# Turning, taking and summing the later units' queries one step later in an attention and two-layer kernel

## The reference

```python
# q, k, v: (4, 8, 576, 64); pooled attention over means of 4 tokens, plus a banded local attention
q_d, k_d, v_d = means of 4 neighbouring tokens
out_up = repeat(softmax(q_d k_d^T / 8) v_d, 4)
out_local = softmax(where(|i - j| < 4, q k^T / 8, -1e9)) v
x = (out_up + out_local) as (2304 tokens, 512)
g = s * max(x @ w_in, 0)**2 + b        # 512 x 2048
x = g @ w_out                          # 2048 x 512
out = ((x @ w_a) * (x @ w_b)) @ w_out2 # 512 x 1536, 1536 x 512
```

## Time and profile before

| what | value |
|---|---|
| time, median of 3 runs | 975.58 us (975.18 to 975.60) |
| the profiled execution's own time | 975.64 us |
| its span, first to last instruction | 973.8 us |
| TensorE matmuls, busy | 951.3 us (98% of the span) |
| VectorE, ScalarE, GpSimd, busy | 611.1, 474.5, 202.0 us (63%, 49%, 21%) |
| granted TensorE clock, mean | 0.984 |
| DMA, mean over the span | 73 GB/s |

### The profile page before, as it was taken

How to read it: one execution, slowest core, us unless ns; L and a number is a source line. 1 busy time by engine, 2 the same in 40 slices (tenths; PEclk the granted TensorE clock), 3 DMA queues, 4 the chain that set the end, 5 groups by cost and what they waited for, 6 DMA issues and landing times.

```text
span 973.8 us, 18322 instructions
## 1 busy us (share of the span) xinstructions
PE 951.3 (98%) x6902; PEld 898.5 (92%) x6902; DVE 611.1 (63%) x1087; ACT 474.5 (49%) x1112; POOL 202.0 (21%) x216
## 2 busy tenths in 40 slices
PE   6899999999999999999999999999999999999997
PEld 5799999999999999999999999999999999999996
DVE  5788655655555556555547666666856667766642
ACT  4677554545554445454434544444634345644432
POOL 2200211001210011200012033333333333333310
PEclk8599999999999999999999999999999999999999
DMA  8346220111300122101041142222442222422201
GB/s 199 104 136 164 65 59 20 45 45 43 88 21 20 48 64 67 44 19 44 14 154 34 50 137 66 66 66 66 135 143 79 67 66 66 130 66 65 75 24 66
DMA packets 129352, 71.41 MB, mean 73 GB/s; under 512 B 63248, under 2 KB 120304, under 8 KB 129264
## 3 DMA queue, kind: packets, MB, share of 16 engines
q1 hardware_dynamic: 128224, 69.94, 25.0%
q10 hardware_dynamic: 1040, 0.29, 0.1%
HBM read 60.76 MB, written 9.44 MB: 72 GB/s over the span
## 4 chain that ended last, share of the span: by engine, by line
PE 88%; ACT 6%; DVE 3%; issue 2%; DMA 1%; SPq 1%; POOL 0%; ACTq 0%; DVEq 0%
PE bank L736 27%; PE bank L686 19%; PE bank L672 18%; PE bank L752 15%; ACT sml L795 3%; PE bank L572 2%; PE bank L636 2%; PE bank L619 1%; PE bank L629 1%; PE bank L548 1%; DMA natk<-in_k 1%; ACT smp L786 1%; PE bank L603 1%; PE bank L566 1%; ACT kT L774 1%
## 5 line engine op out<-in xcount | busy, mean ns | idle before, releaser
L736 PE MATMUL bank<-wx 128*128 128x384 f32 x1512 | 287.4, 336 | 0.6 <-ACT u L977 0.6
L736 PEld LDWEIGHTS bank<-wx 128*128 128x128 f32 x1512 | 267.1, 188 | 14.6 <-ACT u L977 0.9
L686 PE MATMUL bank<-g_hi,wx 128*128 128x288 f32 x1024 | 232.1, 302 | 0.0
L672 PE MATMUL bank<-wx 128*128 128x288 f32 x1536 | 226.9, 296 | 0.5 <-ACT relu L889 0.5
L672 PEld LDWEIGHTS bank<-wx 128*128 128x128 f32 x1536 | 211.7, 189 | 0.7 <-ACT relu L889 0.7
L1236 POOL TENSOR_TENSOR raw<-raw 128x256 f32<-128x256 f32 x144 | 143.3, 1013 | 302.9 <-DVE wx L1156 263.4
L686 PEld LDWEIGHTS bank<-g_hi,wx 128*128 128x128 f32 x1024 | 171.4, 188 | 5.3 <-issue 5.2
L752 PE MATMUL bank<-wx 128*128 128x512 f32 x648 | 173.4, 394 | 0.8 <-DVE wx L1156 0.8
L686 PE MATMUL bank<-g_lo,wx 128*128 128x288 f32 x512 | 151.5, 296 | 0.0
L752 PEld LDWEIGHTS bank<-wx 128*128 128x128 f32 x648 | 119.3, 188 | 17.2 <-DVE wx L1156 1.5
L1112 DVE SCALAR_TENSOR_TENSOR g_lo<-relu,b_col,g_hi 128x288 fp32r<-128x288 f32 x128 | 70.6, 552 | 80.4 <-ACT g_hi L894 80.4
(11 more groups left out here) (70 smaller groups left out, 858.8 us busy)
## 6 DMA issues: line engine op xcount, KB each, us to landing
raw<-in_moe_w_b SPq DMA_DIRECT2D x72, 128.0 KB, 2.3
raw<-in_moe_w_a SPq DMA_DIRECT2D x72, 128.0 KB, 2.3
raw<-in_moe_w_out SPq DMA_DIRECT2D x36, 256.0 KB, 2.8
vnat<-in_v SPq DMA_DIRECT2D x32, 144.0 KB
o_transposed<-o_sb SPq DMA_DIRECT2D x8, 576.0 KB, 3.4
o_raw<-o_transposed SPq DMA_DIRECT2D x6, 768.0 KB, 6.3
out<-y SPq DMA_DIRECT2D x18, 256.0 KB, 2.3
natq<-in_q SPq DMA_DIRECT2D x63, 72.0 KB, 2.1
```

The lines of the kernel that those rows point to most:

```text
L672: mm = nc.tensor.matmul(HB[:, 0:HALF], wi(w, kd, f), xs(x, c % 2)[:, kd], start=(kd == 0 and j == 0), stop=(kd == KD - 1 and j == 2))
L686: mm = nc.tensor.matmul(ACC[o][:, 0:HALF], wo(w, f, o), g[:, slot % GB, :], start=(f == 0 and j == 0), stop=(f == F1 - 1 and j == 2))
L736: mm = nc.tensor.matmul(dst, left(w, n, a, kd), right(x, i)[:, kd * HC:(kd + 1) * HC], start=(opens and kd == 0 and m == 0), stop=(kd == K ...
```

## The change

`turn_q` and `take_q` of units 4 to 31 go from tick -4 to tick -3, `sum_q` from tick -3 to tick -2. The alone units keep their ticks. No instruction, wait or buffer is added or taken away.

```diff
@@ TensorE
-                for u in at_tick(g, 1, -4, TURN_SKEW):
+                for u in at_tick(g, 1, -3, TURN_SKEW):
                     turn_q(u)
@@ VectorE
-                for u in at_tick(g, 2, -3, TURN_SKEW):
+                for u in at_tick(g, 2, -2, TURN_SKEW):
                     sum_q(u)
```

## The result

| | before | with the change |
|---|---|---|
| median | 975.38 us (974.59 to 975.60, 4 runs) | 987.86 us (987.70 to 988.27, 4 runs) |
| ratio | | 1.013 (95% interval 1.0113 to 1.0148) |
| span of the profiled execution | 973.8 us | 985.9 us |

A forecast was written before the change was run, and what follows sets the result against it. TensorE's list was taken to bound the kernel, its matmuls busy for 951.3 of 973.8 us. The terms -3.7 + 5.0 + 4.7 + 1.2 + 1.2 = +8.4 us on 975.6 us gave 984.0 us, range 980.8 to 988.5.

The forecast's parts named there:

- The clock: Rival, 8%: after chunk 0's waits of 2.3 us TensorE falls to 1.2 GHz, 4.2 us a fall: 988.2 or 992.4 us.
- Part 1: Leading units: `turn_q` no longer waits for `take_k`, 0.34 us at each of 11 waits, -3.7 us; no new stall.
- called by 0.06 us: Unit 18, which leads: TensorE reaches `turn_local` at 260.97, where 260.91 would do, so no stall.
- Part 2: Units 12 to 15, 20 to 23, 28 to 31: `turn_local` newly waits 0.42 us each for `take_q`, +5.0 us.
- Part 3: Chunk 0: `take_q` behind two splits of weights delays `turn_local`; units 6 and 7 +4.7 us, unit 8 +1.2 us.
- the short waits vanish inside that one: Unit 8: TensorE's short waits for the keys' transfer and `take_k` vanish, since ScalarE sets the end.
- Part 4: Units 4 and 5: later `take_q` and `sum_q` delay `scores`, then `turn_local`; +1.2 us together, bounds +0.5 and +2.4.
- Against it: the waits are short, and the matmuls before them unbroken: Argument against a fall to 1.2 GHz after chunk 0's waits of 2.3 us; that rival got 8%.
- a low digit in the page's clock row: Sign that the forecast is wrong: the changed kernel's clock row has a low digit behind the second slice.
- the forecast's second ground for it: Transposes, which follow each long wait, do not count as work for TensorE's clock, by the Trainium skill.
- nothing waits: Rival, 6%: `turn_local` finds the queries taken at every unit, only the leading units' gain is left: 971.9 us.
- long waits are handed back: Rival, 6%: waits of 2.35 us in units 6 and 7 spare TensorE later waits, taking off 4.7 us: 979.3 us.

The follow-up runs named there:

- the run filled with transposes: The change plus 22 extra transposes of the identity ahead of `turn_local` of units 5, 6 and 7, results not used: 984.27 us.
- the filled kernel: The change plus 13 extra matmuls into the free bank 1 ahead of `turn_local` of units 5, 6 and 7, results not used: 984.05 us.
- only leading units late: Against the kernel before, `turn_q`, `take_q` and `sum_q` one tick later for the 11 leading units only (9 to 11, 16 to 19, 24 to 27): 971.66 us.
- ahead of the splits: The change with `take_q` of units 5 to 8 on ScalarE behind `split_g_hi` but ahead of the two splits of weights: 978.53 us.

## Why the prediction was right, and where it was short

The direction, the mechanism and the four parts of the sum held. The clock, which had no term in the sum, did not.

- **Part 1, leading units: right.** -3.7 us was forecast; -3.96 by slots, -4.2 in the kernel that has nothing else. The stall was put at 0.34 us, it was 0.36. That no new stall follows there was called by 0.06 us; none shows.
- **Part 2, units that don't lead: right.** +5.0 forecast, +5.07 by slots, 0.42 each as taken.
- **Part 3, the waits of chunk 0: right in size.** 4.7 + 1.2 = 5.9 forecast; 5.75 once the clock is held up. The long part of them is the two splits of weights, as the kernel with `take_q` ahead of them shows. By slots the three cost 2.26, 1.65 and 1.83 us, not 2.35, 2.35 and 1.2. `turn_local` is held as long at unit 7 as at unit 6 (86.62 - 82.60 = 4.02 us from the start of its up group, against 66.82 - 62.79 = 4.03), but some of that comes back before unit 8: the 0.38 us that TensorE waited for the transfer of unit 8's keys, at 91.37, are gone, and the wait for unit 8's queries is longer by as much and more. The forecast had said that the short waits vanish inside that one, so the sum of the two, 3.48 us, is what it gave (3.55).
- **Part 4, units 4 and 5: right, hidden by chance in the table.** +1.2 forecast. From unit 3's `values` (L629) to the third up group it was 50.37 - 38.35 = 12.02 us and is now 50.91 - 37.79 = 13.12, so +1.10. The other profiles repeat this: 12.02 to 12.03 in the four kernels that start as before or move only TensorE's turning there, 13.11 in the four that start as the change does. In the change's profiled execution the start came to L629 0.56 us sooner, hence +0.55 in the table; over the ten profiles that moment lies anywhere from 37.60 to 38.54.
- **The clock: wrong.** This is the step "Against it: the waits are short, and the matmuls before them unbroken". The fall was priced as a rival at 8% and left out of the sum. It came after all three long waits, unit 8's of 1.7 us too, and cost 4.63 us in all, 1.5 us for each. The rival's own price of 4.2 us a fall was too high: I took four groups of matmuls at the low clock, and each low stretch of 3.42 us has room for 1.2 groups of 2.79 us. No row of the trace before had an idle time of this length at full clock, and absence of a row was read as evidence. The forecast's sign for it, a low digit in the page's clock row, could not have shown it either: three stretches of 3.42 us leave every slice of 24.6 us at a 9. The rule of the Trainium skill ("TensorE: Matmul & The Clock Gate", "HAM oscillation — how this bites in real kernels") that idle gaps between bursts lower the clock, which the forecast weighed and did not follow, was the better guide. The trace agrees with it in direction only: the waits in the page's example are longer than the 1.67 to 2.20 us here, and the forecast's second ground for it, that transposes don't count, failed in the run filled with transposes.

The measured 12.5 us are then -3.96 + 5.07 + 5.75 + 1.10 + 4.63 = 12.6. Without the clock it would be 8.0, where the sum had 8.4. That the time still fell inside the range is luck: the range was wide enough for it because it added up high bounds of parts that came out near their middle, not because it foresaw three falls.

The rival *nothing waits* (971.9 us) fell for the change as made, and gives the time of the kernel in which only TensorE's turning is late, 971.77 us, to 0.1 us. The rival *long waits are handed back* fell: the filled kernel keeps 5.75 us of them in slots 4 to 16, and slots 16 to the end show no gain beyond the leading units'.

## What to carry to other kernels

When a step is moved on several engines at once, ask for each whether the move serves anything there: here TensorE's move alone brings 4 us. ScalarE's copy and VectorE's sum, moved along with it, cost 16 us; by the waits most of that is the copy's, which lands behind work that finishes late. Before a copy is put later, compare the tail of what it will stand behind with the moment its reader arrives; two engines that meet within 0.1 us are one small shift away from a stall. And price an idle time of TensorE of 2 us twice: once as a wait, once for the clock.

## What the runs showed of the hardware that was not expected

Waits of 1.67, 2.18 and 2.20 us on a TensorE that had been at full clock for the 17 to 20 us before the fall were each followed by a stretch of 3.42 us at 1.2 GHz, which began 0.2 to 1.5 us after the work had resumed, and so slowed work rather than idle time. Waits of 1.39 and 1.40 us were not, and 2 us of transposes in the same place held the clock up as matmuls did.

In the start the clock rises at different times in kernels whose code is the same there. With only leading units late, whose start is instruction for instruction that of before, the clock is up from 41.95 us on, and the first up group takes 1.74 us:

```profile
41.95:44.00 2.05, 2.05 (x17) 2.04 (x16) 2.05 (x3) 1.30 (x2) 0.00 (x0) 1.00 0.06 13
```

```profile
42.86 1.74 PE L679 MATMUL bank<-wx 128*128 128x288 f32 x12
```

while before it is 0.50 from 40 to 44 us, and that group takes 2.79. The fifth up group starts at 58.95 and 58.86 us all the same: TensorE, sooner at the second up group, waits 1.39 us for ScalarE's relu there instead of 0.51, and the higher clock brings nothing.

The clock's number has a trap. In the profile of *ahead of the splits* the view gives 1.00 for all of the start, yet the first up group takes longer than the 2.79 us of the low clock:

```profile
44.87 3.05 PE L672 MATMUL bank<-wx 128*128 128x288 f32 x12
```

The trace's first clock record lies at 47.74 us, and what comes before it is printed as 1.00. In the start the clock is better read from how long a known group takes.
